# A recurrence in tiles of 128 tokens for both batches in turn, and a first expert layer in blocks of 256 tokens

## The reference, cut to what matters

```python
for t in range(S):                       # S = 768, B = 2, H = 8, D = 40
    m_new = np.maximum(f_gate[:, :, t] + m, i_gate[:, :, t])
    C = exp(f + m - m_new) * C + exp(i - m_new) * outer(v, k)
    n = exp(f + m - m_new) * n + exp(i - m_new) * k
    y[:, :, t] = sigmoid(o) * (C @ q) / max(abs(n @ q), 1)
x = y as (1536, 320)
x = (sigmoid(x @ w_gate) * (x @ w_val)) @ w_out                    # layer one
xn = x / rms(x) * rms_g
out = (silu(xn @ w_gate2) * (xn @ w_val2)) @ w_out2                # layer two
```

## Time and profile before

| | |
|---|---|
| median of three runs | 541.31 us |
| the profiled execution | 541.75 us, of which its span is 540.0 us |
| TensorE busy | 497.2 us, 92% of the span |
| VectorE busy | 323.4 us, 60% |
| ScalarE busy | 180.1 us, 33% |
| GpSimd busy | 66.3 us, 12% |
| chain that ended last | TensorE 81%, VectorE 14%, issue 2%, ScalarE 1% |
| DMA | 28.38 MB, 53 GB/s over the span |

### The profile page before, as it was taken

The page is one execution under the profiler, slowest core; times in us unless marked ns, Lnnn a source line. Parts: engine busy times, 40 slices in busy tenths (PEclk is TensorE's granted clock), DMA queues, the critical chain, the costliest instruction groups (busy, mean ns, idle before and its releaser), DMA issues.

```text
span 540.0 us, 7882 instructions
## 1 busy us (share of the span) xinstructions
PE 497.2 (92%) x2948; PEld 474.6 (88%) x2948; DVE 323.4 (60%) x809; ACT 180.1 (33%) x337; POOL 66.3 (12%) x86
## 2 busy tenths in 40 slices
PE   0987169999999999999999999999999999999997
PEld 0755168999998999989999989999999999999997
DVE  7888949787487874788753574575055315513550
ACT  1365013454135540455413553332123213312320
POOL 5275930000100001000010001720000000000000
PEclk9999999999999999999999999999999999999999
DMA  4663341030310202301320233100000000000001
GB/s 121 171 203 122 124 123 30 1 80 1 103 51 2 78 1 63 93 0 41 84 85 1 89 121 122 36 1 1 33 5 1 12 25 2 0 26 13 0 1 36
DMA packets 28869, 28.38 MB, mean 53 GB/s; under 512 B 14240, under 2 KB 25760, under 8 KB 28832
## 3 DMA queue, kind: packets, MB, share of 16 engines
q1 hardware_dynamic: 28832, 27.89, 17.3%
HBM read 25.92 MB, written 1.97 MB: 52 GB/s over the span
## 4 chain that ended last, share of the span: by engine, by line
PE 81%; DVE 14%; issue 2%; ACT 1%; POOL 0%; DVEq 0%; ACTq 0%
PE bank L858 17%; PE bank L859 17%; PE bank L861 11%; PE bank L875 7%; PE bank L877 7%; PE bank L876 7%; PE bank L814 4%; PE bank L797 3%; DVE cst L608 2%; DVE den L615 2%; PE bank L757 2%; PE bank L816 1%; DVE y_tok L618 1%; PE bank L783 1%; DVE wgv_lo L686 1%
## 5 line engine op out<-in xcount | busy, mean ns | idle before, releaser
L858 PE MATMUL bank<-x_hi,wgv_hi 128*128 128x384 f32 x576 | 199.2, 346 | 2.3 <-DVE x_lo L626 1.2
L859 PE MATMUL bank<-x_lo,wgv_hi 128*128 128x384 f32 x576 | 193.6, 336 | 0.0
L861 PE MATMUL bank<-x_hi,wgv_lo 128*128 128x384 f32 x384 | 129.2, 336 | 0.0
L858 PEld LDWEIGHTS bank<-x_hi,wgv_hi 128*128 128x128 f32 x576 | 108.9, 189 | 4.7 <-DVE wgv_hi L687 1.7
L859 PEld LDWEIGHTS bank<-x_lo,wgv_hi 128*128 128x128 f32 x576 | 109.0, 189 | 1.4
L464 ACT ACTIVATE h_hi<-hf 128x384 fp32r<-128x384 f32 x96 | 50.4, 525 | 151.6 <-DVE hf L707 151.6
L875 PE MATMUL bank<-wo_hi,h_hi 128*128 128x320 f32 x288 | 91.9, 319 | 0.5 <-DVE hf L707 0.5
L877 PE MATMUL bank<-wo_hi,h_lo 128*128 128x320 f32 x288 | 89.0, 309 | 0.0
L876 PE MATMUL bank<-wo_lo,h_hi 128*128 128x320 f32 x288 | 89.0, 309 | 0.0
L705 DVE TENSOR_TENSOR sg<-sg,bank 128x384 f32<-128x384 f32 x48 | 26.6, 554 | 98.1 <-PE bank L859 90.4
L861 PEld LDWEIGHTS bank<-x_hi,wgv_lo 128*128 128x128 f32 x384 | 72.6, 189 | 0.0
(11 more groups left out here) (143 smaller groups left out, 563.8 us busy)
## 6 DMA issues: line engine op xcount, KB each, us to landing
raw<-in_w_gv SPq DMA_DIRECT2D x16, 576.0 KB, 4.1
raw<-in_w_o SPq DMA_DIRECT2D x8, 480.0 KB, 3.3
y<-y_tok SPq DMA_DIRECT2D x12, 160.0 KB, 1.8
step_a<-in_k_t SPq DMA_DIRECT2D x7, 180.0 KB
step_a<-in_q_t SPq DMA_DIRECT2D x7, 180.0 KB
step_a<-in_v_n SPq DMA_DIRECT2D x7, 160.0 KB
step_a<-in_k_n SPq DMA_DIRECT2D x7, 160.0 KB
step_a<-in_o_g SPq DMA_DIRECT2D x7, 160.0 KB
```

Source lines behind the costliest of these rows:

```text
L858: pe.matmul(ps[:, 0:TOK], wgv_hi[:, w, k, cs], x_hi[:, k, xs], start=(k == 0), stop=False)
L859: mm = pe.matmul(ps[:, 0:TOK], wgv_hi[:, w, k, cs], x_lo[:, k, xs], start=False, stop=(k == 2))
L861: pe.matmul(ps[:, 0:TOK], wgv_lo[:, w, k, cs], x_hi[:, k, xs], start=False, stop=False)
```

## The change

The recurrence now takes both batches in turn: tile n is tokens 128*(n//2) on of batch n % 2. The gates of all 16 rows (2 batches x 8 heads) and 768 tokens are loaded at once; the rows are worked out in three parts, token tile 0, tile 1, and tiles 2 to 5 (`PARTS`). Ahead of the first step of layer one only tiles 0 and 1 are done. D now puts even heads in one bank and odd heads in the next; S is 8 matmuls of 128 columns over 40 rows, from rows 0 or 64 in turn; the combination N takes all heads at once (`combine`), and the state is updated apart (K: one product on VectorE, two instructions on GpSimd). GpSimd also builds `d_rhs` from tile 2 on and `vk`. The transposes of layer one's output (O) are woven into the next block.

Layer one goes in 6 blocks of 256 tokens (tiles 2k and 2k+1), with the recurrence of tiles 2k+2 and 2k+3 woven in; layer two stays at 4 blocks of 384. Layer one's weights are rounded on ScalarE and split on GpSimd beside the first block: chunks 0 and 1 ahead of it, chunk c of the rest after the step that `SPLIT_AT` gives. Layer two's gate and value weights are split in the same way beside block 5, its output weights after it (rounded on ScalarE, the low parts on GpSimd).

```diff
+FIRST = [[("K", 0), ("A", 1, 0), ("A", 1, 1)], [("K", 1), ("A", 1, 2), ("B", 2)], [("D", 2), ("R", 1), ("B", 3)],
+         [("S", 2)], [], [("N", 2), ("K", 2)], [("D", 3), ("A", 2, 0)], [("S", 3), ("T", 2)], [("A", 2, 1)],
+         [("N", 3), ("K", 3)], [("A", 2, 2)], [("T", 3)], [], [("R", 2), ("B", 4)], [], [("B", 5)]]
+def woven(k):
+    a, b = 2 * k + 2, 2 * k + 3
+    slots = [[] for _ in range(16)]
+    slots[1] += [("O", 2 * k - 2)]
+    slots[3] += [("O", 2 * k - 1)]
+    if k < NB0 - 1:
+        slots[0] += [("D", a)]
+        slots[2] += [("S", a)]
+        slots[4] += [("N", a)]
+        slots[5] += [("D", b)]
+        slots[6] += [("S", b), ("T", a)]
+        slots[8] += [("N", b)]
+        slots[10] += [("T", b)]
+        if k < NB0 - 2:
+            slots[5] = [("K", a), *slots[5]]
+            slots[8] += [("K", b)]
+            slots[11] += [("B", a + 2)]
+            slots[13] += [("B", b + 2)]
+SPLIT_AT = {0: [2], 1: [3], 2: [4], 3: [5], 4: [6], 5: [7], 7: [8], 8: [9], 9: [10], 10: [11]}
...
 def _(pool):
+            def split_gv(lay, c):
+                pool.wait_ge(whi, c + 1)
+                pool.tensor_tensor(wgv_lo[:, c, :, :], r[:, 0:2, :], wgv_hi[:, c, 0:2, :].bitcast(F32), ...)
+                pool.wait_ge(wlo, c + 1)
+                pool.tensor_tensor(wgv_hi[64:P, c, 2, :], r[64:P, 2, :], wgv_hi[64:P, c, 2, :].bitcast(F32), ...)
...
+                if kind == "B":
+                    pool.wait_ge(rows_done, min(n // B, len(PARTS) - 1) + 1)
+                    pool.wait_ge(d_done, 2 * (n - B) + 2)
+                    pool.tensor_tensor(d_rhs[b][0:Q + R, :, :, :], l_row ..., sel ..., ALU.mult).then_inc(drhs_p, 1)
+                elif kind == "S" and n < NT - B:
+                    pool.tensor_tensor(heads(vk[b]), heads(va[b]), el ..., ALU.mult).then_inc(vk_done, 1)
+                elif kind == "K" and n >= B:
+                    pool.wait_ge(n_done, n + 1)
+                    link(pool.tensor_tensor(heads(cst[b][:, :]), heads(cst[b][:, :]), gcol ..., ALU.mult))
+                    pool.wait_ge(cn_done, n + 1)
+                    pool.tensor_tensor(cst[b][:, :], cst[b][:, :], cnew[:, :], ALU.add).then_inc(cst_done, 1)
...
 def _(act):
+            for k in range(NB0):
+                for slot in range(NF + 4):
+                    if slot < NF:
+                        sigmoid(0, NF * k + slot, slot)
+                        h_high(0, NF * k + slot, slot)
+                    for what in WEAVE[k][slot]:
+                        piece(what)
+                    if k == 0:
+                        for c in SPLIT_AT.get(slot, []):
+                            high(0, c)
+                    if k == NB0 - 1 and slot < NF and slot % FC == FC - 1:
+                        high(1, 2 * (slot // FC))
+                        high(1, 2 * (slot // FC) + 1)
...
 def _(dve):
+            for sub in range(3):
+                rows(0, sub)
+            diagonal(0)
+            diagonal(1)
+            for kind in "SNT":
+                for n in range(B):
+                    piece((kind, n))
+            def combine(n):
+                dve.wait_ge(n_done, n + 1)
+                if j:
+                    link(dve.tensor_tensor(heads(inter), heads(bank[7]), ecol ..., ALU.mult))
+                    dve.tensor_tensor(num[:, :], inter[:, :], src, ALU.add).then_inc(num_done, 1)
+                dve.tensor_scalar(den[:, :], heads(src)[:, :, D], 1.0, None, ALU.max)
+                link(dve.tensor_tensor(heads(o_sig[b]), heads(src)[:, :, 0:D], heads(o_sig[b]), ALU.mult))
+                link(dve.scalar_tensor_tensor(den[:, :], heads(src)[:, :, D], -1.0, den[:, :], ALU.mult, ALU.max))
+                link(dve.reciprocal(rden[:, :], den[:, :]))
+                link(dve.tensor_tensor(heads(y[:, 0:DM]), heads(o_sig[b]), rden ..., ALU.mult))
+                dve.tensor_copy(y[:, DM:3 * P], y[:, 2 * P:DM]).then_inc(y_done, 1)
...
+            for k in range(NB0):
+                for slot in range(NF + 4):
+                    if slot < NF:
+                        gate(0, NF * k + slot, slot)
+                        if slot:
+                            h_low(0, NF * k + slot - 1, slot - 1)
+                    for what in WEAVE[k][slot]:
+                        piece(what)
...
 def _(pe):
+                if kind == "D":
+                        pe.wait_ge(drhs_p, n - B + 1)
+                        pe.wait_ge(cn_done, min(n, NT - B))
...
+                elif kind == "S":
+                    pe.wait_ge(e_done, 2 * n + 2)
+                    for c in range(4):
+                        for i in range(2):
+                            rs = slice(64 * i, 64 * i + D)
+                            mm = pe.matmul(bank[base(n) + i][:, c * P:(c + 1) * P], sq[b][rs, 1, c, :], sq[b][rs, 0, c, :],
+                                           start=True, stop=True)
...
             def hidden(lay, k, f, halves=(0, 1)):
+                    elif f >= 2:
+                        pe.wait_ge(hf_done, n - 1)
+                    if k == 0 and i == 0:
+                        pe.wait_ge(split0, 2 * (c + 1))
+            for kind in "DSNT":
+                for n in range(B):
+                    piece((kind, n))
+            for k in range(NB0):
+                for slot in range(NF + 4):
+                    if slot < NF:
+                        hidden(0, k, slot)
+                    else:
+                        project(0, k, *divmod(slot - NF, 2))
+                    for what in WEAVE[k][slot]:
+                        piece(what)
```

More of the change, by code:

```diff
@@ L36, with mlstm_moe_kernel @@
 EPS = 1.0e-6
-UNITS = BT * NG
-STEP_DMAS = 8
-ALONE = [*(("A", part) for part in range(5)), ("B", 0), ("D", 0), ("B", 1), ("S", 0, 0), ("R",), ("S", 0, 1),
[3 rows of a table removed]
-WOVEN = [[("A", 0)], [("A", 1)], [("A", 2)], [("A", 3), ("A", 4)], [("B", 0)],
[5 rows of a table removed]
[L54 to L85, removed]
+N0 = B * P
+NB0 = NJ
+T1 = 3
+N1 = T1 * P
+NB1 = NT // T1
+F1 = NB0 * NF
+PARTS = [(0, 1), (1, 2), (2, NJ)]
+FIRST = [[("K", 0), ("A", 1, 0), ("A", 1, 1)], [("K", 1), ("A", 1, 2), ("B", 2)], [("D", 2), ("R", 1), ("B", 3)],
[19 more added lines that the diff above has]
+            slots[13] += [("B", b + 2)]
+    return slots
+WEAVE = [FIRST, *(woven(k) for k in range(1, NB0))]
+SPLIT_AT = {0: [2], 1: [3], 2: [4], 3: [5], 4: [6], 5: [7], 7: [8], 8: [9], 9: [10], 10: [11]}
+def mlstm_moe_kernel(nc, gates, qk_t, q_t, vok, w_gv, w_o, rms_g, out):
     ctx = ExitStack()
@@ L101, in mlstm_moe_kernel @@
         wo_lo = sb("wo_lo", [P, NF, DM], F32R)
[L102 to L112, removed]
+        raw_p = sb("raw_p", [P, 3 * CW], F32)
@@ L312, in _ @@
+            for t in range(T1):
+                sp.wait_ge(out_sent[t], 16 * NB1)
         @block.gpsimd
@@ new lines, in piece @@
+            def piece(what):
+                kind, n, *more = what
+                if kind == "A":
+                    rows(n, *more)
+                elif kind == "S":
+                    weigh(n)
+                elif kind == "N":
+                    combine(n)
+                elif kind == "K":
+                    update(n)
+                elif kind == "T":
+                    dve.wait_ge(xh_done, n + 1)
+                    dve.tensor_tensor(x_lo[:, n, :, :], t_view(bank[base(n) + 2]), x_hi[:, n, :, :].bitcast(F32),
+                                      ALU.subtract).then_inc(x_done, 1)
+                elif kind == "O":
+                    dve.wait_ge(xh2_done, n + 1)
+                    dve.tensor_tensor(x_lo[:, n, :, :], t_view(bank[7]), x_hi[:, n, :, :].bitcast(F32),
+                                      ALU.subtract).then_inc(x2_done, 1)
@@ L752, in _ @@
+            for k in range(NB1):
+                for f in range(NF):
+                    n = F1 + NF * k + f
+                    gate(1, n, f)
+                    if f:
+                        h_low(1, n - 1, f - 1)
+                    if k == 0 and f in (1, 3):
+                        piece(("O", NT - B + f // 2))
+                h_low(1, F1 + NF * k + NF - 1, NF - 1)
         @block.tensor
         def _(pe):
-            def turn(slot, ps):
-                for k in range(3):
-                    mm = pe.transpose(t_view(ps)[:, k, :], y_tok[:, slot, k * P:(k + 1) * P], ident[:, :])
-                mm.then_inc(t_done, 1)
@@ new lines, in piece @@
+            def piece(what):
+                kind, n, *_ = what
+                b = n % B
+                j = n // B
+                if kind == "D":
+                    if n < B:
+                        pe.wait_ge(drhs_v, n + 1)
+                        pe.wait_ge(selc_done, n + 1)
+                        pe.wait_ge(consts, 3)
+                    else:
+                        pe.wait_ge(drhs_p, n - B + 1)
+                        pe.wait_ge(cn_done, min(n, NT - B))
+                        pe.wait_ge(p_done, 2 * n)
+                    for i in range(2):
+                        dp = bank[base(n) + i]
```

1269 lines of the change are left out of this document (625 added, 644 removed), and 8 rows, old and new, of tables (ALONE, WOVEN).

## The result

The changed kernel takes 529.26 us (median of 4 runs, 525.22 to 529.83) against 541.37 (540.68 to 541.91): a ratio of 0.9754, interval 0.9708 to 0.9799, so 2.5% faster where 0.7% was forecast. Run again beside the experiments it took 528.64 (ratio 0.9768, 0.9750 to 0.9786). The profiled execution is the fastest, 525.22 us for a span of 523.5; its terms stand against the 536.0 of the forecast.

What follows compares the result with a forecast made beforehand. TensorE bounds layer one's blocks and layer two, after a 72.9 us start. 31.0 + 68.5 + 3 x 50.0 + 48.5 + 36.5 + 201.5 = 536.0, 537.3 on the median's footing, against 541.3; range 521 to 554.

Steps and rivals of the forecast that it cites:

- Part 1, the start: Before the first hidden matmul: only tiles 0 and 1 are left, taking 31.0 us instead of 72.9; bounds 28 and 35.
- rival B: S's matmuls from rows 0 and 64 overlap, saving 8 pass times in each of 12 tiles: 525 us, chance 0.12.
- TensorE is at half speed here: In the start: TensorE runs at 1.2 GHz, 384 columns starting 0.32 us apart against 0.174 later.
- Part 2, (a): First block, T its first matmul: slot 3 waits for chunk 3 until T+17.7, behind rows and GpSimd; matmuls there at T+9.5.
- Part 2, (b): First block: VectorE, slowed beside GpSimd, reaches h_low(11) at T+64.6; 6.3 us of projection follow, T+71; 68.5 taken for the block.
- the ties: First block: GpSimd was let go first whenever it tied with VectorE; 2.5 us were taken off for that, giving 68.5.
- the walk: First block followed slot by slot for its waits; without any loss to GpSimd it gives 58 us.
- Part 3, woven blocks: Blocks 1 to 3 of layer one: 49.6 us of TensorE work, 50.0 taken for each; bounds 48.5 and 53.
- a late table load: Woven blocks: the second tile's S waits for exponentials behind ScalarE's 1.28 us table load, 0.8 late.
- Part 4 and 5: Block 4 at 48.5 us, block 5 at 36.5 (bounds 35 and 41); layer two at 201.5 against 200.3 before.
- A: Rival: the first block runs without loss to GpSimd, 58 us, and the start at 30; 526 us, chance 0.20.
- C: Slower rival: loss to GpSimd strikes every block of layer one, 3.5 us a block for four blocks; 556 us, chance 0.26.

Runs made afterwards that it cites:

- early rows: The changed kernel with VectorE computing the second part of the rows ahead of the first gate, and GpSimd building tile 2's right operand one slot earlier: 521.44 us.
- both, without low parts: Changed kernel with second-part rows ahead of the first gate, third part cut in two, and layer one's low parts zeroed by memsets: 516.21 us, ratio 0.9547.

## Why the prediction was right, and where it was not

The direction and the mechanism were right: the start pays, the first block takes the largest part back, the rest is TensorE's. The size came out of errors that partly cancelled.

- **Part 1, the start (31.0, measured 23.6).** D started at 8.5 instead of 9.5, since VectorE began at 0.9 and not at the 2.1 of before, and took 3.2 instead of 3.4. S took 2.1 instead of 6.8, N with a wait in it 4.7 instead of 6.2, and the rest 5.1, as forecast. The largest error is S, and it has two parts. At half rate throughout S takes 3.79 us (the start with early rows), so 3.0 of the 4.7 are the overlap of rows 0 and 64, which the forecast had put aside as rival B. The other 1.7, and the 1.5 of N, are the step "TensorE is at half speed here": true of almost all of D in every profile and of one whole start, but here full rate came with D's last pair. The forecast took the clock of one execution of before for a property of the stage; the same code has starts of 23.6 to 27.3.
- **Part 2, (a).** Step 3 forecast at T+17.7, measured T+17.5; removing the wait gave 5.5 us by step 3. Right in place and price.
- **Part 2, (b).** The last `h_low` was forecast at T+64.6 and landed at T+64.1. The lock is shown by the run without it: 8.0 us, where the forecast had 68.5 - 58 = 10.5 (13 before the ties). Two terms of the sum were off. The 2.5 us taken off for ties was not there. And the rest of the projection was priced at 6.3 us at full rate, but took 9.0: after TensorE's wait of 4.16 us its matmuls stood 0.27 us apart until 93.0, and 0.147 only from there. In the one run that has no wait there (both, without low parts) they ran at full rate from the first. 2.5 and 2.7, less the 0.5 by which `h_low` was early, make the block's 4.6 but for rounding. The agreement at T+64 is luck. Without loss the walk had the last `h_low` at T+51.7 (58 - 6.3); with memsets in the place of the subtractions it landed at T+55.7. The loss on top was 12.9 in the forecast and is 8.4. Two errors of some 4 us cancelled.
- **Part 3, woven blocks (50.0, measured 47.7 to 47.9).** 256 columns at 0.120: right. The tile at 8.0: measured about 7.05 ((47.73 - 23.0 - 10.6)/2). S, 1.16 us in place of 1.8, is 0.64 of the 0.95; no run separates the rest. That is rival B's mechanism, to which the forecast gave 0.12. Its price in the start held (3.0 of its 3.4), in the woven blocks it was too high: five of a tile's eight overlaps undone cost 0.54 us a block of two tiles, since one tile hides its part in a wait for VectorE. The 0.4 us that the forecast added for a late table load are not there. The Trainium skill, page TensorEngine Tiling (Array Packing), section "Key Properties", which says that different tiles can load weights and multiply in parallel, was the better guide here than the rows of same-row products; the traces agree, with 7 and 105 ns in turn against 107 to 112 for each.
- **Part 4 and 5.** Block 4 carries the error of the woven blocks (46.1 for 48.5). Block 5 36.7 for 36.5. Layer two 200.6: of the 1.2 us added for ScalarE's rounding and two transposes 0.3 appeared; no run separates them.
- **The rivals.** A fell (no loss to the lock): the loss is 8 us, and with memsets in its place the block still takes 65.1 and not 58. C fell: no woven block is over 47.9, and moving GpSimd's work out of `h_low`'s way there changes nothing. The forecast argued against C by VectorE's 20 idle us in a block, and the runs bear that out (24.3 idle in block 1).
- **Slips in the numbers.** C charges block 4 with 10 us of GpSimd, which by part 4 has no K and no B. The chance of faster comes to 0.57, not 0.58. The earlier trace rows give 0.10 us a pass, not 0.11; the later traces give 0.11.

**Better versions.** Rows of block 1 early, with the last part where VectorE idles (519.32 us) or with an earlier right-hand side (518.89 us), beat the change by some 10 us and the kernel before by 4%; their intervals overlap, so the two cannot be ranked.

## What to carry to other kernels

Price a lock between two engines in the stages in which the slower one is waited for, and nowhere else: here it cost 8 us in the first block, and in the three woven blocks with K and B, moving one of GpSimd's two right-hand sides off an `h_low` gained nothing. Before moving in-order work to another stage, read that engine's idle stretches there and put it into them: the same 6.8 us of VectorE work cost 4.9 us ahead of three gates and 0.8 in the gaps (of the difference, up to 1.6 may be TensorE's clock). Do not carry the clock level of one execution of a short, broken stage over to the next kernel; give it a range. And where a clock column and the distances between matmuls disagree, believe the distances.

## What the hardware showed that I had not expected

- Two float32 products with operands of 40 rows, one at row 0 and one at row 64, overlap: their passes start in twos, 7 ns apart, every 112 ns, where passes from the same rows stand 107 to 112 ns apart one by one, with weights loaded for each.
- The same code for the start takes 23.6, 26.1 or 27.3 us. With TensorE at half rate to the end S takes 3.79 us and N 7.05; with full rate from D's last pair on they take 2.06 and 4.68.
- After a wait of 4.16 us TensorE did 9.79 us of dense work at a mean granted clock of 0.68, 3.0 us more than the 6.74 of the same 42 matmuls where it had not waited.
